# GpSimd's low-part subtraction of each weight chunk in four instructions of 256 columns

## The reference

```python
# mixture: mask = tokens given to expert e (greedy, at most N // E = 384 each)
h = np.maximum(x[mask] @ w1[e], 0.0)
out[mask] = h @ w2[e]
# last stage, for all tokens
h = x @ w_in
e = np.exp(h - np.max(h, axis=-1, keepdims=True))
solu = h * (e / (np.sum(e, axis=-1, keepdims=True) + 1e-09))
mu = np.mean(solu, axis=-1, keepdims=True)
var = np.mean((solu - mu) ** 2, axis=-1, keepdims=True)
return ((solu - mu) / np.sqrt(var + 1e-06) * g_ln) @ w_out
```

## Time and profile before

| | |
|---|---|
| median of three runs | 861.91 us |
| the profiled execution | 860.36 us, of which its span is 858.6 us |
| mean granted TensorE clock | 0.925 of full speed |
| PE busy | 719.1 us (84%) |
| DVE busy | 550.8 us (64%) |
| GpSimd busy | 335.8 us (39%) |
| ACT busy | 317.9 us (37%) |
| L1292, 60 of the 64 subtractions | 155.7 us, 2595 ns each |

### The profile page before, as it was taken

One profiled execution on the slowest core, in us unless ns is written; L12 is line 12 of the kernel. 1 busy time (PEld: TensorE's weight loads), 2 busy tenths in 40 slices (PEclk: granted clock), 3 DMA queues, 4 the chain that ended last, 5 costly groups with the idle time before them and its releaser, 6 DMA issues.

```text
span 858.6 us, 18982 instructions
## 1 busy us (share of the span) xinstructions
PE 719.1 (84%) x6837; PEld 620.4 (72%) x6838; DVE 550.8 (64%) x2135; ACT 317.9 (37%) x521; POOL 335.8 (39%) x243
## 2 busy tenths in 40 slices
PE   4768858311998999999998999999899989989993
PEld 3546646201896989789887988797898879888982
DVE  3434634686878677877787696878787876823140
ACT  2223424002314631462355146414623551473160
POOL 5790000007524740672175147406712750573001
PEclk9787978655899999999999999999999999999997
DMA  8987963005103311330132033113202320331000
GB/s 346 355 301 256 368 221 123 15 0 176 57 1 111 99 50 50 99 98 25 61 111 74 25 105 116 49 49 99 98 25 65 107 74 25 110 112 48 1 13 37
DMA packets 24935, 89.16 MB, mean 104 GB/s; under 512 B 3360, under 2 KB 3360, under 8 KB 24864
## 3 DMA queue, kind: packets, MB, share of 16 engines
q0 software_dynamic: 14208, 50.34, 17.8%
q1 hardware_dynamic: 10656, 37.97, 12.4%
HBM read 75.71 MB, written 12.58 MB: 103 GB/s over the span
## 4 chain that ended last, share of the span: by engine, by line
PE 60%; DVE 11%; issue 11%; POOL 8%; DMA 6%; ACT 2%; DVEq 0%; ACTq 0%; POOLq 0%; SPq 0%
PE bank L503 16%; PE bank L504 14%; PE bank L505 14%; POOL wl L1292 6%; DMA raw<-w,w_idx 4%; PE bank L436 3%; PE bank L393 2%; PE banks L418 2%; PE bank L403 2%; DMA unit<-unit_in 2%; PE bank L429 2%; DVE hits L958 1%; DVE hot_b L1039 1%; DVE z L1087 1%; PE banks L532 1%
## 5 line engine op out<-in xcount | busy, mean ns | idle before, releaser
L1286 POOL DMA_INDIRECT raw<-w,w_idx x60 | 59.4, 990 | 286.9 <-DVE w_idx L1007 249.6
L1292 POOL TENSOR_TENSOR wl<-raw,wh 128x1024 fp32r<-128x1024 f32 x60 | 155.7, 2595 | 26.1 <-ACT wh L729 24.8
L729 ACT ACTIVATE wh<-raw 128x1024 fp32r<-128x1024 f32 x60 | 63.4, 1056 | 92.7 <-DMA raw<-w,w_idx 92.6
L503 PE MATMUL bank<-xh,wh 128*128 128x384 f32 x256 | 91.3, 357 | 3.7 <-DVE xl L1133 3.4
L503 PE MATMUL bank<-hh,wh 128*128 128x384 f32 x256 | 90.1, 352 | 0.0
L505 PE MATMUL bank<-xh,wl 128*128 128x384 f32 x256 | 86.9, 340 | 0.0
L504 PE MATMUL bank<-xl,wh 128*128 128x384 f32 x256 | 86.9, 340 | 0.0
L505 PE MATMUL bank<-hh,wl 128*128 128x384 f32 x256 | 86.0, 336 | 0.0
L504 PE MATMUL bank<-hl,wh 128*128 128x384 f32 x256 | 85.9, 336 | 0.0
L503 PE MATMUL bank<-wout_h,uh 128*128 128x512 f32 x192 | 80.2, 417 | 0.0
L503 PE MATMUL bank<-win_h,yh 128*128 128x512 f32 x192 | 77.3, 402 | 0.0
(11 more groups left out here) (178 smaller groups left out, 1613.7 us busy)
## 6 DMA issues: line engine op xcount, KB each, us to landing
unit<-unit_in SPq DMA_DIRECT2D x24, 768.0 KB, 6.5
unit<-unit_in SPq DMA_DIRECT2D x24, 520.0 KB, 5.6
x_rows<-x_sb SPq DMA_DIRECT2D x24, 256.0 KB, 4.7
raw<-w_in POOLq DMA_DIRECT2D x4, 512.0 KB, 8.5
raw<-w_out POOLq DMA_DIRECT2D x4, 512.0 KB, 6.2
raw<-w,w_idx POOLq DMA_INDIRECT x60, 4.2
gath<-x_rows,ids POOLq DMA_INDIRECT x24, 3.7
out<-z,ids_prev POOLq DMA_INDIRECT x14
```

What stands on the lines that cost most here:

```text
L503: nc.tensor.matmul(bank, stat_h, mov_h, start=first, stop=False)
L729: nc.scalar.activation(wh[:, c % WCH, :], stage(s, c), ACT.Copy).then_inc(w_hi, 1)
L1286: gp.indirect_dma_start(stage(s, c), None, table, bass.IndirectOffsetOnAxis(ap=w_idx[:, c % WCH:c % WCH + 1], axis=0))\
L1292: gp.tensor_tensor(wl[:, c % WCH, :], stage(s, c), wh[:, c % WCH, :].bitcast(F32), ALU.subtract)\
```

## The change

`weight_lo` issues four subtractions of 256 columns each, in place of one of 1024. Only the last of the four counts up `w_ready`. The same function serves all 64 chunks.

```diff
+LO_PIECES = 4
...
             def weight_lo(s, c):
                 gp.wait_ge(w_hi, 2 * WCH * s + (c + 1))
-                gp.tensor_tensor(wl[:, c % WCH, :], stage(s, c), wh[:, c % WCH, :].bitcast(F32), ALU.subtract)\
-                  .then_inc(w_ready, 1)
+                for q in range(LO_PIECES):
+                    cols = slice(1024 // LO_PIECES * q, 1024 // LO_PIECES * (q + 1))
+                    lo = gp.tensor_tensor(wl[:, c % WCH, cols], stage(s, c)[:, cols], wh[:, c % WCH, cols].bitcast(F32),
+                                          ALU.subtract)
+                lo.then_inc(w_ready, 1)
```

## The result

The changed kernel takes 872.92 us (median of 17 runs, 867.96 to 881.84) against 862.88 us of the kernel before in the same sessions: ratio 1.0122, 95% interval 1.0099 to 1.0145. It is slower by about 10 us; the forecast was 877 us with a range of 862 to 890. The profiled execution has a span of 875.0 us and a mean granted clock of 0.909, so it is 16.4 us longer than the profiled one of before, more than the medians differ. What is read from these two alone has to be taken with care; the pair of profiles in experiment 5, both near full clock in the experts, is the better one to compare.

A forecast was written before the change was run, and what follows sets the result against it. GpSimd, through raw 6 behind wl 4, was taken to set when PE goes on. The profiled 860.36 us plus 13.2 us of lateness and 4.3 us of TensorE's clock made 877.9, forecast as 877 us, range 862 to 890.

The forecast's parts named there:

- What three more instructions cost a chunk: GpSimd's subtraction of each chunk: three added instructions at 0.14 us each, 0.42 us a chunk, ends 0.12 and 2.7 us.
- What it gives DVE and costs GpSimd at wl 0: Where z(0) meets wl 0: z(0) ends 1.5 us sooner, some 0.3 us remain at xl; wl 0 takes 1.15 us more.
- Raw 6 later, 1.6 us per passage in experts 2 to 6: GpSimd's DMA raw 6 behind wl 4: 1.6 us later, delaying ACT, ul and PE; five experts, 8.0 us.
- the slack ahead of wl 3: GpSimd's wait for wh 3 ahead of wl 3: taken as 1.28 us in experts 2 to 6, absorbing that much delay.
- Expert 1, +1.3 us: Passage of expert 1: with its slack of 1.56 us ahead of wl 3, 1.3 us longer.
- Expert 7, +3.5 us: Passage of expert 7: no slack, z(1) meets wl 2, four of five subtractions count; 3.5 us longer.
- TensorE's clock, +4.3 us: Half clock behind PE's longer waits in experts 2 to 6: 1.7 us each, half of five counted, +4.3 us.
- The step from 877.9 to 877: Final adjustment: the profiled execution lies 1.55 us below the median; the sum of 877.9 us became a forecast of 877.
- DVE shut out: Rival at wl 0: pieces follow so closely that DVE does not get in between; 870 us, chance 0.16.
- Nearly free: Rival on GpSimd's pieces: 0.04 us each, 0.12 us a chunk, no clock loss; 863 us, chance 0.15.
- dearer pieces: Rival on GpSimd's pieces: 0.25 us each, 0.75 us a chunk; about 889 us, chance 0.12.
- Faster: Rival at wl 0 and wl 3: DVE's z is served in openings between pieces; 853 us, chance 0.09.

The follow-up runs named there:

- experiment 5: Five unread matmuls added in each of PE's two waits per passage: changed kernel 866.95 us, ratio 1.0052; kernel before 854.36 us, 0.9925.
- filled pair: Profiles of the changed kernel and the kernel before, both with five unread matmuls in each of PE's two waits per passage: 865.7 and 853.0 us.
- experiment 4: wh 6 made behind uh on ACT in experts 1 to 7: changed kernel 858.17 us, ratio 0.9962; kernel before 853.66 us, 0.9912.
- experiment 6: Kernel before with DVE's loop over experts 1 to 6 written out: 851.54 us, ratio 0.9878; also with wh 6 behind uh: 847.66 us, 0.9835.

## Why the prediction was right, and where it was not

- *What three more instructions cost a chunk.* Forecast 0.42 us, measured 0.40 with four pieces and 0.97 for seven more with eight. The short comparison in the earlier trace rows, 0.14 us to the next start, was the right row; the power instruction of the earlier trace rows would have misled by more than six times. The prediction's estimate from the Trainium skill's figure, up to 0.9 us, was twice too high.
- *What it gives DVE and costs GpSimd at wl 0.* z(0) fell by 2.2 us, not 1.5: it did its work at once, and the first piece was held up (1.89 us), instead of the other way round. wl 0 paid 1.15 us, as forecast from wl 3. Of z(0)'s gain 0.34 us were left behind `xh` (forecast 0.3), and the turn of DVE's loop ate these, too. This the prediction had not seen, though the row with its 2.36 us was there.
- *Raw 6 later, 1.6 us per passage in experts 2 to 6.* At full clock raw 6 was 1.1 us later and the passage 1.2 us longer (filled pair), with the slack ahead of wl 3 gone as forecast (1.31 us) and z(1) giving back 0.5 (it still met wl 3, but had begun 0.4 us ahead of it). In the unfilled profiles raw 6 of expert 5 was 1.7 us later, near the forecast by luck: 0.91 us of the slack stayed, because wh 3 stands behind an `hh` that PE, at half clock, delivers later. That raw 6 is coupled to PE was right (experiment 4). What failed is "for PE, since PE already waits there": the wait at the transposes did not grow in either pair of profiles, it fell. The delay had reached PE earlier in the passage, at wh 4, by way of `hh`, `hl` and the count. The prediction had set 2.3 us as the bound under which raw 6 would not bind as it was read; expert 5 lies below it (2.19), experts 3, 4 and 6 at 2.4.
- *Expert 1, +1.3 us.* It had the wrong sign: 1.3 us less in the filled pair, where the clock was 1.0 with pieces and 0.96 without, and 1.5 us less in the unfilled one (77.34 against 78.80 us from z(0) to z(0)) at 0.96 in both. There PE waits directly for the rows' low part `xl`, behind expert 0, which is not in the loop: 3.40 us before and 1.57 us with pieces, filled. It is the one place where the sooner z(0) reaches PE.
- *Expert 7, +3.5 us.* Right: z(1) met wl 2 as described, which took 3.80 us there. From the start of wl 0 to the issue of raw 6 it is 25.5 us (757.73 to 783.18) against 22.4 before (743.93 to 766.32), 3.1 us more. The filled pair's 3.3 us hold some clock as well (0.95 against 1.00 over these stretches).

```profile
769.40 3.80 POOL L1295 TENSOR_TENSOR wl<-raw,wh 128x256 fp32r<-128x256 f32 x4
...
783.18 0.96 POOL L1287 DMA_INDIRECT raw<-w,w_idx  x1 [0.81 <-POOL wl L1295]
```

- *TensorE's clock, +4.3 us.* This is the term that failed: filled waits gave both kernels the same, 0.70 and 0.75 per cent, so no net cost of the clock could be shown. The spells came in the profiled execution, though behind waits of 2.2 us and not of 3.8. That the kernel before has them too in its ordinary executions is inferred from those gains; if so, they were counted against a baseline that was one lucky profile. Without this term the sum is 860.4 + 13.2 = 873.6, next to the measured 872.9; that is partly luck, since the passages and expert 1 brought some 5 us less than forecast (8.4 of 13.2), and the medians of before lie 1.5 to 2.5 us above the profiled run. The step from 877.9 to 877 had no ground: for a median the 1.55 us were to be added, not taken off.

The rivals: DVE shut out (870 us) was near in time and wrong in mechanism, as z(0) went to 1.22 us. Nearly free and dearer pieces are both ruled out by the 0.40 us. Faster is ruled out: where z(0) meets wl 0, the chunk still pays 1.15 us.

What stays open is how the 1.2 per cent divides between the two paths in the changed kernel itself. Experiment 4 says half to half, but its ratios have intervals of 0.3 per cent each, and with one path removed the other has more to bind; the waits of the filled pair put the added time at the counts. Open, too, is what share the clock has, within the 0.5 per cent either way that experiment 5 leaves.

## What to carry to other kernels

When an instruction on a shared port is cut up so that another engine gets in sooner, price three things apart: the fixed part of each added instruction, the time that the cut one now gives away, and who was really waiting for the engine that gains. Here the engine that gained (DVE) had its gain taken by `xh`, for which it had to wait anyway, and by its loop's turn, while the one that lost (GpSimd at 39% busy) stood on PE's path through the fixed orders of ACT and DVE. A single profile can be a lucky one in its clock: a loss seen in it has to be tried on the kernel before as well. And slack ahead of a wait counts only as long as what is waited for comes no later: here PE's clock moved wh 3, and 0.91 of 1.44 us of slack stayed unused.

## What the runs showed of the hardware

- GpSimd: a two-input subtraction of 1024, 4 x 256 and 8 x 128 columns takes 2.41, 2.81 and 3.38 us, so 0.13 to 0.14 us for each instruction more, though the instructions overlap in the record.
- An indirect DMA issue on GpSimd that meets DVE's z ended 0.84 us after z did, wherever it began: 0.28 us before z's end (raw 2 of expert 5 before, 1.12 us), 0.6 us before it (expert 7 before, 1.44 us), or 0.22 us ahead of z's start, with z(1) at 595.45 for 1.21 us in the kernel of experiment 6 with wh 6 behind uh. There it took 2.27 us instead of 0.96.

```profile
595.23 2.27 POOL L1288 DMA_INDIRECT raw<-w,w_idx  x1 [0.82 <-POOL wl L1294]
```

- The turn of DVE's loop shows 1.8 to 3.0 us of idle time, and more of it when DVE arrives sooner (10.9 us in five turns before, 13.8 after). Written out, the kernel is 1.2 per cent faster.
- Unread matmuls in waits of 2 us gave 0.7 per cent in both kernels.
